# A third PSUM bank for the feed-forward products, and the attention's transposes and value products regrouped

## The reference

```
attn: 8 heads of 64; softmax(q k^T / 8 + mask) v; heads 0-3: the 32 last keys,
      heads 4-7: every 4th of the 128 last keys
ff:   xk, xr = mixes of x with x shifted by one token
      out = sigmoid(xr @ w_r) * (relu(xk @ w_k)**2 @ w_v)          (512 -> 1024 -> 512)
mlp2: u = x + (relu(x^T @ w_tok1) @ w_tok2)^T                      (tokens 576 -> 256 -> 576)
      out = u + relu(u @ w_ch1) @ w_ch2                            (512 -> 1536 -> 512)
```

## Time and profile before

| what | value |
|---|---|
| median of 3 runs | 736.88 us (736.03 to 736.9) |
| the profiled execution's own time | 736.99 us |
| its span, first to last instruction | 735.2 us |
| PE busy | 717.6 us, 98% of the span, 6463 matmuls |
| DVE, ACT, POOL busy | 370.6, 257.6, 224.5 us |
| granted clock of PE | 0.999 |
| phase 1 and 2 | up to about 362 us, and from there |

### The profile page before, as it was taken

The page is one execution under the profiler, slowest core; times in us unless marked ns, Lnnn a source line. Parts: engine busy times, 40 slices in busy tenths (PEclk is TensorE's granted clock), DMA queues, the critical chain, the costliest instruction groups (busy, mean ns, idle before and its releaser), DMA issues.

```text
span 735.2 us, 15645 instructions
## 1 busy us (share of the span) xinstructions
PE 717.6 (98%) x6463; PEld 691.5 (94%) x6463; DVE 370.6 (50%) x629; ACT 257.6 (35%) x628; POOL 224.5 (31%) x237
## 2 busy tenths in 40 slices
PE   8989999999999999999999999999999999999997
PEld 7869899999999999999999999999999999999997
DVE  6588867586776767576741224512245122441222
ACT  4585463635444453636341112311123111231111
POOL 5497654756464664735036000000000000000000
PEclk9999999999999999999999999999999999999999
DMA  9931333222322320100912010300103001010021
GB/s 209 278 73 34 59 66 67 46 55 45 59 55 45 54 57 20 50 21 1 361 47 66 1 33 9 89 2 1 33 5 93 1 1 33 5 29 1 1 33 33
DMA packets 127190, 39.89 MB, mean 54 GB/s; under 512 B 116168, under 2 KB 120720, under 8 KB 127120
## 3 DMA queue, kind: packets, MB, share of 16 engines
q1 hardware_dynamic: 122864, 33.39, 20.4%
q0 software_dynamic: 1088, 4.72, 1.9%
q10 hardware_dynamic: 3168, 0.79, 0.6%
HBM read 29.43 MB, written 4.72 MB: 46 GB/s over the span
## 4 chain that ended last, share of the span: by engine, by line
PE 83%; DVE 7%; POOL 4%; issue 2%; ACT 2%; DMA 1%; DVEq 0%; POOLq 0%; ACTq 0%
PE bank L755 14%; PE bank L756 13%; PE bank L757 13%; PE tq L755 4%; PE tq L757 4%; PE tq L756 4%; PE bank L1225 4%; PE bank L1224 3%; PE s L1225 3%; PE bank L1223 3%; PE s L1223 3%; PE s L1224 3%; PE bank L677 3%; PE bank L641 2%; PE s L549 2%
## 5 line engine op out<-in xcount | busy, mean ns | idle before, releaser
L1200 DVE SCALAR_TENSOR_TENSOR h_lo<-tq,h_hi 128x288 fp32r<-128x288 f32 x48 | 22.0, 458 | 114.1 <-ACT h_hi L1196 114.1
L1200 DVE SCALAR_TENSOR_TENSOR h_lo<-bank,h_hi 128x288 fp32r<-128x288 f32 x48 | 22.0, 458 | 113.4 <-ACT h_hi L1196 113.4
L755 PE MATMUL bank<-k_hi,WV_hi 128*128 128x288 f32 x256 | 78.0, 305 | 0.0
L756 PE MATMUL bank<-k_hi,WV_lo 128*128 128x288 f32 x256 | 75.5, 295 | 0.0
L757 PE MATMUL bank<-k_lo,WV_hi 128*128 128x288 f32 x256 | 75.3, 294 | 0.0
L755 PE MATMUL bank<-xk_hi,WK_hi 128*128 128x288 f32 x224 | 69.1, 308 | 5.0 <-DVE kr L818 4.4
L756 PE MATMUL bank<-xk_hi,WK_lo 128*128 128x288 f32 x224 | 66.1, 295 | 0.0
L757 PE MATMUL bank<-xk_lo,WK_hi 128*128 128x288 f32 x224 | 65.9, 294 | 0.0
L833 POOL TENSOR_TENSOR k_lo<-kr,k_hi 128x288 fp32r<-128x288 f32 x64 | 55.8, 876 | 24.3 <-ACT k_hi L829 23.6
L866 DVE RECIPROCAL rg<-rg 128x288 f32<-128x288 f32 x32 | 61.3, 1920 | 3.0 <-ACT rg L855 3.0
L1196 ACT ACTIVATE h_hi<-tq 128x288 fp32r<-128x288 f32 x48 | 19.8, 412 | 122.3 <-PE tq L757 122.3
(11 more groups left out here) (185 smaller groups left out, 2142.4 us busy)
## 6 DMA issues: line engine op xcount, KB each, us to landing
C_raw<-in_moe_w_ch SPq DMA_DIRECT2D x6, 1024.0 KB, 11.4
xcur<-X POOLq DMA_DIRECT2D x4, 1152.0 KB, 5.8
out_x<-blocks SPq DMA_DIRECT2D x112, 36.0 KB, 1.7
vt<-in_v SPq DMA_DIRECT2D x40, 80.0 KB, 2.4
qraw<-in_q SPq DMA_DIRECT2D x128, 24.0 KB, 1.9
kraw<-in_k SPq DMA_DIRECT2D x128, 24.0 KB, 1.9
vt<-in_v SPq DMA_DIRECT2D x7, 320.0 KB, 3.4
WK_raw<-in_moe_w_k SPq DMA_DIRECT2D x4, 512.0 KB, 8.6
```

The source lines that it names most:

```text
L755: e.matmul(out_ap, wh, xh, start=start and i == 0, stop=False)
L756: e.matmul(out_ap, wl, xh, start=False, stop=False)
L1200: e.scalar_tensor_tensor(lo, ps, 0.0, hi.bitcast(F32), ALU.max, ALU.subtract).then_inc(Z.h2l_done, 1)
```

## The change

From unit 1 on the feed-forward products rotate over three banks instead of two: `bank0`, `bank1` and the upper half of `tq2`. Product g then waits for product g - 3; in unit 1 the first three products have waits of their own. For blocks from n = 8 on, the second half of the transposed probabilities goes to the lower half of `tq2`, no longer to `p_ps`, and both halves are transposed at step t + 7 and copied out at the head of step t + 8. The value products get a list `values` of their own at the very end of a step; for blocks 9 to 22 they stand in the step in which the scores of block n + 1 stand, behind these. For blocks at place A that is one step earlier than before, and for B and C the same step with the order of the two turned round. The transposes of X at the end of phase 1 go to the halves of `s2`, and the first token products, which stay in `tq2`, get two waits: for the copies of the last probabilities and for the 31st `x2_done`.

```diff
--- before.py
+++ after.py
@@ -618,7 +618,9 @@
 
         def p_bank(n, h):
 
-            return (p_ps, mlp_ps[1], mlp_ps[0])[(2 * n + h) % 3] if n < 4 else p_ps
+            if n < 4:
+                return (p_ps, mlp_ps[1], mlp_ps[0])[(2 * n + h) % 3]
+            return tq2[:, 0:512] if n >= NPE and h else p_ps
 
         def p_buffer(n):
             return pTs[n] if n < 4 else pT
@@ -635,8 +637,12 @@
                 if n < 4:
                     before, half = divmod(2 * n + h - 3, 2)
                     wait(e, Z.ptb_done if half else Z.pta_done, before + 1)
+                elif n < NPE:
+                    e.wait_ge(Z.pta_done if h else Z.ptb_done, n + h)
+                elif n == NPE:
+                    e.wait_ge(Z.q_done if h else Z.ptb_done, n)
                 else:
-                    e.wait_ge(Z.pta_done if h else Z.ptb_done, n + h)
+                    e.wait_ge(Z.ptb_done if h else Z.pta_done, n)
                 for g in range(4):
                     last = e.transpose(ps[0:KB, TR * g:TR * (g + 1)], sb[0:TR, GC * h + KB * g:GC * h + KB * (g + 1)],
                                        ident[0:TR, 0:TR])
@@ -762,7 +768,12 @@
 
         def bank_free(e, hh, kind, i):
 
-            g = SEQ.index((kind, i)) - 2
+            back = 3 if hh else 2
+            g = SEQ.index((kind, i)) - back
+            if hh == 1 and g == -1:
+                return e.wait_ge(Z.k_done, NPE)
+            if hh == 1 and g < 0:
+                return e.wait_ge(Z.x2_done, DT + g + 2)
             if g < 0:
                 return wait(e, Z.x2_done, DT * hh + g + 1)
             k_, n = SEQ[g]
@@ -773,8 +784,12 @@
             else:
                 e.wait_ge(Z.x2_done, DT * hh + n + 1)
 
-        def ff_bank(kind, i, n):
-            return mlp_ps[SEQ.index((kind, i)) % 2][:, 0:n]
+        def ff_bank(hh, kind, i, n):
+
+            g = SEQ.index((kind, i))
+            if hh == 0:
+                return mlp_ps[g % 2][:, 0:n]
+            return (mlp_ps[0][:, 0:n], mlp_ps[1][:, 0:n], tq2[:, 512:512 + n])[(HP * (hh - 1) + g) % 3]
 
         def product_number(hh, kind, i):
             return HP * hh + SEQ.index((kind, i)) + 1
@@ -786,7 +801,7 @@
 
             n = FU[hh][2]
             j = FT1 * hh + f
-            ps = ff_bank("k", f, n)
+            ps = ff_bank(hh, "k", f, n)
             t = tile(kr, j % NKR, n)
 
             def tensor(e):
@@ -836,7 +851,7 @@
         def gate(hh, d):
 
             n = FU[hh][2]
-            ps = ff_bank("r", d, n)
+            ps = ff_bank(hh, "r", d, n)
 
             def tensor(e):
                 bank_free(e, hh, "r", d)
@@ -869,7 +884,7 @@
         def down(hh, d, part):
 
             b, t0, n = FU[hh]
-            ps = ff_bank("v", d, n)
+            ps = ff_bank(hh, "v", d, n)
 
             def tensor(e):
                 if part == 0:
@@ -966,6 +981,7 @@
             early = [[] for _ in range(UNITS * NU)]
             main_ = [[] for _ in range(UNITS * NU)]
             late = [[] for _ in range(UNITS * NU)]
+            values = [[] for _ in range(UNITS * NU)]
             for n, t in enumerate(STARTS, 4):
                 if n < NPE:
                     late[t].append(transposes(n))
@@ -980,10 +996,11 @@
                 late[t + 5].append(normalise(n))
                 late[t + 7].append(p_transpose(n, 0))
                 early[t + 8].append(p_evict(n, 0))
-                late[t + 8].append(p_transpose(n, 1))
-                early[t + 9].append(p_evict(n, 1))
-                late[t + 9].append(weighted_values(n))
-                early[t + 10].append(x_evict(n))
+                late[t + (8 if n < NPE else 7)].append(p_transpose(n, 1))
+                early[t + (9 if n < NPE else 8)].append(p_evict(n, 1))
+                tv = STARTS[n - 3] + 2 if NPE < n < ND - 1 else t + 9
+                values[tv].append(weighted_values(n))
+                early[tv + 1].append(x_evict(n))
             for i in range(4):
                 late[i].append(split_wr(i))
             for hh in range(NU):
@@ -1008,7 +1025,7 @@
                 hi, lo = split_wk(i)
                 late[5 + i].append(hi)
                 late[(8, 8, 10, 9, 12, 11, 14, 13)[i]].append(lo)
-            return [e + m + x for e, m, x in zip(early, main_, late)]
+            return [e + m + x + v_ for e, m, x, v_ in zip(early, main_, late, values)]
 
         def load_x(b):
 
@@ -1047,12 +1064,12 @@
             tt = XSEQ[i]
             tail = tt == NTT - 1
             nt = S - TT * tt if tail else P
-            ps = work[2 + i % 2] if first else work_bank(b - 1, "x", i)
+            ps = acc[i % 2] if first else work_bank(b - 1, "x", i)
 
             def tensor(e):
                 if first:
                     if i == 0:
-                        e.wait_ge(Z.k_done, ND)
+                        e.wait_ge(Z.masked, ND)
                         e.wait_ge(Z.x2_done, DT * 2)
                     elif i >= 2:
                         e.wait_ge(Z.xtl_done, i - 1)
@@ -1100,6 +1117,9 @@
                     if not first:
                         for m_ in range(2):
                             work_free(e, b - 1, "t1", m_)
+                    else:
+                        e.wait_ge(Z.ptb_done, ND)
+                        e.wait_ge(Z.x2_done, DT * NU - 1)
                     e.wait_ge(Z.xtl_done, NTT * (b + 1))
                     e.wait_ge(Z.w_lo2, N_T)
                     t0 = DM * (NTT - 1)
```

## The result

The changed kernel takes 729.38 us (median of 4 runs, 728.01 to 729.79) against 736.85 (4 runs): a ratio of 0.9898, 95% interval 0.9881 to 0.9915, or 7.5 us. The forecast was 729.6. The profiled execution of the changed kernel is 729.79 us long, with a span of 728.0.

A forecast was written before the change was run, and what follows sets the result against it. PE, booked for 98% of 735.2 us, was taken to bound the kernel. The terms 5.75 + 1.0 + 1.2 - 0.5 = 7.4 us, taken from 736.99, gave 729.6 us, with an 8 in 10 range of 728.0 to 733.0.

The forecast's parts named there:

- place A: Group of PE's transposes, scores and values, met five times: 2.95 us of work to become 2.75, 0.20 less each.
- The bank's stalls: Units 2 to 6: PE's five waits for the squaring, 1.15 us each, all gone with three banks, 5.75 us.
- The last unit: Transposes of X: two stalls, 0.66 and 0.34 us, go with three banks, 1.0 us.
- The regrouping: Transposes in rows of eight and scores directly before values save PE 1.2 us together; bounds 2.2 to -0.6.
- The unseen order: Scores, then values after a product, absent from the trace: priced at 1.97 us, kept at 1.9 to 2.1.
- What comes back at place C: Transposes of blocks 11, 14, 17, 20, 23 wait for POOL's normalisation: 0.1 us each, 0.5 in all, within 0 to 2.7.
- Rival 1: PE waits for the normalisation in five blocks, 2.7 us instead of 0.5, time 731.8 us; chance 0.20.
- the 0.49 us of DVE ahead of the mask: DVE's idle wait for the scores of block 11; the mask can move up by at most that.
- The prediction's dearer end: Upper end of the normalisation wait, 0.54 us per block: shifted DVE instructions meet POOL elsewhere and stretch anew.
- edits costed at nothing: Five edits priced at zero, among them both probability copies together in ACT's queue and earlier values with 0.8 us cover.
- rival 2: PE loses the same 1.05 us at the seventh or eighth product; gain only 1.9, time 735 us; chance 0.06.
- rival 3: Values of all 14 pairs wait for ACT's copies; slower, 740.8 us at 0.8 a pair, 747.8 at 1.3; chance 0.02.

The follow-up runs named there:

- e2_regroup_only: Changed kernel with two product banks in every unit, leaving only transposes and values regrouped; 733.48 us, ratio 0.9952 to the kernel before.
- e4_values_apart: Changed kernel with the values of place A one step later again, apart from the scores; 730.74 us, ratio 0.9914 to the kernel before.
- e3_values_first: Changed kernel with the values before the scores in the 14 steps that hold both; 731.70 us, ratio 0.9930 to the kernel before.
- e1_bank_only: Kernel before plus only the third product bank; transposes, copies and values of the probabilities as before; 734.29 us, ratio 0.9961.
- e7_bank_and_second_p: Kernel before plus the third product bank and the second probability bank, halves and values at their old steps; 732.63 us, ratio 0.9952.

## Why the prediction was right

**The bank's stalls.** 5.75 us were to go in units 2 to 6 and did: no wait for the squaring is left. The margin of the seventh product held: the squaring that it needs ended at 133.70 + 0.40 = 134.10 and the product started at 135.91, 1.8 us where the forecast had 1.4. But the term is not the third bank's alone: with two banks and the regrouping it was 5 x 0.76 (e2_regroup_only), because the softmax sums stand ahead of that squaring in DVE's queue and came sooner.

**The last unit.** 1.0 forecast, 35.28 - 34.23 = 1.05 measured, the same in every kernel with three banks and absent in e2_regroup_only.

**The regrouping.** Its 1.2 us was a sum of PE's own prices, and 1.2 is what e2_regroup_only leaves when the shorter stalls are taken off. The unseen order cost 1.98 against an assumed 1.97; that was taken from its nearest row and not worked out. Place A's 0.20 is the 0.20 by which e4_values_apart lengthened the units. The rule of the Trainium skill that the prediction cites (TensorEngine Tiling (Array Packing), section Key Properties: a change of tiling mode drains the engine) fits: the order inside the pair changed the price by 0.01, and one change of mode less at place A saved 0.2. No run separates the drain from other costs of such a change.

**What comes back at place C.** 0.5 forecast; start to start 0.06 ahead of the transposes and (0.86 - 0.78) in the whole row, five times, is 0.4. Rival 1 was no fancy: it is what e3_values_first shows, 0.60 instead of 0.19, and 2.1 us in all by the units, against the 2.2 it was priced at. The forecast chose between the two by one bracket, the 0.49 us of DVE ahead of the mask, and that bracket decided. How near it was, the working did not say. The normalisation had to come 0.39 + 0.05 = 0.44 us sooner for the wait to vanish, and against the kernel before it came (134.06 - 123.28) - (133.86 - 123.55) = 0.47 us sooner; PE came sooner too (135.12 - 123.55 = 11.57 us into its unit, and 134.91 - 123.28 = 11.63 before without the stall), and a wait of 0.06 stayed. The 0.1 us per block was a choice inside 0 to 0.54, and that it fits so well is in part luck.

Two readings behind that choice were off. The mask moved ahead by more than the bound of 0.49: (126.96 - 123.28) - (126.59 - 123.55) = 0.64 us. And only POOL worked back to back between the subtraction and the normalisation's last wait; DVE, which the forecast put beside it, stood idle for 0.52, 0.79 and 0.29 us there, waiting for ACT twice and for POOL once.

The prediction's dearer end cites the rule of the Trainium skill (SBUF — State Buffer, section Who interferes with whom) that a DVE instruction with two SBUF inputs contends with a GpSimd instruction that reads SBUF. The mixes in the lines above still take 0.51 to 1.41 us, and one of the shifted chain's did get longer (1.13 us at 129.74, 0.75 at its place in e3_values_first). It did not hold the chain: in both kernels the next mix then waited for POOL. Of 0.57 us that the mask and the subtraction moved ahead between e3_values_first and the changed kernel, 0.40 arrived at the softmax sums, and the rest was lost on POOL, ahead of its next low part. That needs ACT's `k_hi`, which is tied to PE's product and ended at 129.22 + 0.44 = 129.66; POOL's subtraction had ended at 128.34 + 1.26 = 129.60, and POOL went on at 129.74. In e3_values_first `k_hi` was done before the subtraction, and POOL went on at once. This is read from the two timelines; no run takes ACT's part away.

**Where the working was incomplete.** The second bank of the probabilities stood in the forecast under edits costed at nothing, as a question of ACT's load. Without it five waits of 0.31 us appear once PE is faster (e1_bank_only, e7_bank_and_second_p), 1.5 us that no term named. It did not spoil the sum, since the change contains the cover. Nor does the sum say that its terms depend on each other: by the units the bank alone gains 2.9 us and the regrouping alone 3.2, together 7.5, 1.4 more than their sum.

**The rivals.** The bank wait did not move on (rival 2), and the values did not wait for ACT (rival 3): at place A of block 12 the second copy ended at 150.70 and the values, with the scores ahead of them, began at 152.31, 1.6 us of cover where the forecast had 0.8. The copies were done 150.70 - 149.14 = 1.6 us after their transposes began and not 2.4, since the four of them stand 0.21 to 0.23 us apart.

**The sum.** With what the runs showed for each term it is 5.75 + 1.05 + 1.2 - 0.5 = 7.5 us, and 7.5 was measured. The terms hold for the whole change only: the third bank alone brings two new waits (e1_bank_only), and the regrouping alone already takes a third off the first term (e2_regroup_only).

## What to carry to other kernels

When a stall goes, look at what the waiting engine would meet next at its earlier arrival, and compare times, not shares: here a normalisation 0.7 us ahead of its reader became 0.4 us late. An idle bracket on the engine that feeds that chain tells whether the chain can move up. Here the way to move it was the order of two pieces of work on PE, the engine that bounds the kernel, at no price for PE itself.

Price small matmul groups by start-to-start distances around them, including entry and exit, and measure repeated stages by their own length: 0.1 us in a unit showed clearly where 0.5 us in the whole time did not.

## What the runs showed that was not expected

ACT's copy out of the single probability bank became a stall although ACT is busy for only 49% of the time between 82 and 360 us in e1_bank_only. It stood behind a relu that waits 0.28 us for POOL, in the same place of the unit as in the kernel before, and PE came to it sooner: the queue's order passes a wait for a `kr` buffer on to a bank that has nothing to do with it, 0.31 us each time. That the relu's wait is the cause is read from the timeline; what removed the stall was a second bank (e7_bank_and_second_p).

And giving unit 0's waits a whole step of 1.7 us more cost 2.3 us by the medians (731.17 against 728.90), 2.1 by the lengths of units 0 and 1, instead of saving 3.2.
